# Three of twelve ReLU tiles of each position-bias round move to GpSimd

## The reference

```python
pos = np.arange(S)                                   # S = 576
psi_rel = np.log1p(np.abs(pos[:, None] - pos[None, :]))
psi_i = np.log1p(np.maximum(pos[:, None], 1.0))
x = (psi_rel / psi_i)[..., None]
h = np.maximum(x @ w1 + b1, 0.0)                     # S x S x 32 hidden units
bias = h @ w2                                        # S x S x 8 heads
scores = scores + bias.transpose(2, 0, 1)[None]      # then softmax, times v
```

## Time and profile before

| | |
|---|---|
| timed runs | 1266.56, 1266.70, 1267.24 us; median 1266.7 |
| span of the profiled execution | 1264.6 us |
| bias stage: first VectorE tile to last | 5.02 to 63.84 us |
| first matmul of the attention | 67.56 us |
| DVE busy in the span | 725.5 us (57%), TENSOR_SCALARs at L222: 108 |
| POOL busy in the span | 497.8 us (39%) |
| PE busy in the span | 1219.2 us (96%) |

### The profile page before, as it was taken

How to read it: one execution, slowest core, us unless ns; L and a number is a source line. 1 busy time by engine, 2 the same in 40 slices (tenths; PEclk the granted TensorE clock), 3 DMA queues, 4 the chain that set the end, 5 groups by cost and what they waited for, 6 DMA issues and landing times. The chain is left out here.

```text
span 1264.6 us, 26124 instructions
## 1 busy us (share of the span) xinstructions
PE 1219.2 (96%) x9106; PEld 1096.9 (87%) x9106; DVE 725.5 (57%) x1764; ACT 526.9 (42%) x1188; POOL 497.8 (39%) x588
## 2 busy tenths in 40 slices
PE   6789999999979999999999999999999999999998
PEld 2266777777669999999999999999999999999998
DVE  8977777777779777878778788552112020211111
ACT  6977777777723434344444433212212121212111
POOL 3056666666666424344243444551111111111111
PEclk9989999999999999999999999999999999999999
DMA  5844425252135000000000002340000000000000
GB/s 183 248 146 136 141 95 160 92 179 66 64 95 147 2 1 0 0 0 1 0 0 0 0 0 67 92 117 20 1 19 19 0 19 0 19 0 19 0 19 19
DMA packets 47590, 69.06 MB, mean 55 GB/s; under 512 B 3744, under 2 KB 28480, under 8 KB 47552
## 3 DMA queue, kind: packets, MB, share of 16 engines
q1 hardware_dynamic: 47552, 68.60, 17.4%
HBM read 53.25 MB, written 15.34 MB: 54 GB/s over the span
## 5 line engine op out<-in xcount | busy, mean ns | idle before, releaser
L817 PE MATMUL banks<-x_high,w_high_rest 128*128 128x288 f32 x992 | 293.3, 296 | 0.5 <-PEq L1010 0.5
L818 PE MATMUL banks<-x_low,w_high_rest 128*128 128x288 f32 x992 | 292.8, 295 | 0.0
L819 PE MATMUL banks<-x_high,w_low_rest 128*128 128x288 f32 x992 | 291.8, 294 | 0.0
L1372 DVE TENSOR_TENSOR product<-angle_or_silu,banks 128x288 f32<-128x288 f32 x96 | 43.4, 452 | 312.2 <-PE banks L819 312.2
L1391 POOL TENSOR_TENSOR product_low<-product,product_high 128x288 fp32r<-128x288 f32 x96 | 77.6, 808 | 356.4 <-ACT product_high L1332 356.4
L1190 POOL TENSOR_TENSOR product_low<-product,product_high 128x288 fp32r<-128x288 f32 x128 | 110.4, 863 | 242.5 <-ACT product_high L1070 242.5
L817 PE MATMUL bank<-product_high,w_high_rest 128*128 128x288 f32 x672 | 201.3, 300 | 3.5 <-POOL product_low L1391 2.0
L819 PE MATMUL bank<-product_high,w_low_rest 128*128 128x288 f32 x672 | 197.8, 294 | 0.0
L818 PE MATMUL bank<-product_low,w_high_rest 128*128 128x288 f32 x672 | 197.7, 294 | 0.0
L819 PEld LDWEIGHTS banks<-x_high,w_low_rest 128*128 128x128 f32 x992 | 186.7, 188 | 0.0
L817 PEld LDWEIGHTS banks<-x_high,w_high_rest 128*128 128x128 f32 x992 | 185.9, 187 | 0.7 <-issue 0.7
(11 more groups left out here) (97 smaller groups left out, 2539.4 us busy)
## 6 DMA issues: line engine op xcount, KB each, us to landing
raw_qk<-in_qk SPq DMA_DIRECT2D x32, 576.0 KB, 3.7
bias_scratch<-bias_stage SPq DMA_DIRECT2D x36, 288.0 KB, 3.1
bias<-bias_scratch SPq DMA_DIRECT2D x32, 288.0 KB, 3.1
w_raw<-in_w_out SPq DMA_DIRECT2D x28, 256.0 KB, 2.6
values<-in_v SPq DMA_DIRECT2D x16, 320.0 KB, 4.0
w_raw<-in_w_in SPq DMA_DIRECT2D x16, 256.0 KB, 2.9
out_t<-X SPq DMA_DIRECT2D x7, 576.0 KB, 3.0
w_raw<-in_w_gate SPq DMA_DIRECT2D x12, 256.0 KB, 3.0
```

The source lines that it names most:

```text
L817: nc.tensor.matmul(out, high, x_high, start=start, stop=False)
L818: nc.tensor.matmul(out, high, x_low, start=False, stop=False)
L819: return nc.tensor.matmul(out, low, x_high, start=False, stop=stop)
L1372: dve.tensor_tensor(s[:, :], silu[:, :], val_ps[f % 2][:, 0:NT], ALU.mult).then_inc(s_ready, 1)
```

## The change

GpSimd makes the last tile (j = 3, `POOL_STEP`) of each of the three groups of a round, in VectorE's form. ScalarE makes two tiles of k = 0 instead of three (`ACT_STEPS = [2, 0, 0]`). VectorE makes what is left: one tile of k = 0 (j = 2), three of k = 1, three of k = 2. ScalarE's three copy-outs of a round stay, and so does the shift, whose cut follows `ACT_STEPS`. TensorE has one more wait before each group. GpSimd's rounds are written out one by one; its two prepares come after its tiles of rounds 1 and 2 instead of ahead of everything.

```diff
-    ACT_STEPS = [3, 0, 0]
+    ACT_STEPS = [2, 0, 0]
+    POOL_STEP = STEPS - 1
...
             att.setup(pool)
-            att.prepare(pool, 0, 0)
-            att.prepare(pool, 0, 1)
+            pool.wait_ge(slope_ready, 2)
+            pool.wait_ge(table_in, 16)
+
+            def groups(n, parity, step):
+                for k in range(KINDS):
+                    back = 1 if k == KINDS - 1 else 2
+                    if step >= back:
+                        pool.wait_ge(bias_summed[k], n + 1 - back)
+                        after_waits(pool, pool_passed)
+                    pool.tensor_scalar(hidden[parity][k][POOL_STEP][:, :], table_window(n, k, POOL_STEP),
+                                       slope_of(n, k, POOL_STEP), neg_b1[:, :], ALU.mult, ALU.max
+                                       ).then_inc(pool_hidden[k], 1)
+
+            for n in range(N):
+                groups(n, n % 2, min(n, 2))
+                if n in (1, 2):
+                    att.prepare(pool, 0, n - 1)
...
-                for j in range(ACT_STEPS[0]):
+                for j in range(KINDS):
                     if step > 1 and j == 0:
                         act.wait_ge(bias_summed[0], n - 1)
-                    act.activation(hidden[parity][0][j][:, :], table_window(n, 0, j), ACT.Relu, bias=b1c,
-                                   scale=slope_of(n, 0, j)).then_inc(act_hidden[0], 1)
+                    if j < ACT_STEPS[0]:
+                        act.activation(hidden[parity][0][j][:, :], table_window(n, 0, j), ACT.Relu, bias=b1c,
+                                       scale=slope_of(n, 0, j)).then_inc(act_hidden[0], 1)
                     if step > 0:
                         stage_out(n - 1, 1 - parity, j, step <= 2)
...
-                    for j in range(ACT_STEPS[k], STEPS):
+                    for j in range(ACT_STEPS[k], POOL_STEP):
...
                     pe.wait_ge(dve_hidden[k], n + 1)
+                    pe.wait_ge(pool_hidden[k], n + 1)
```

More of the change, by code:

```diff
@@ L105, in bias_phase @@
     dve_hidden = [sem_of(f"p0_dve_hidden{k}") for k in range(KINDS)]
+    pool_hidden = [sem_of(f"p0_pool_hidden{k}") for k in range(KINDS)]
     bias_summed = [sem_of(f"p0_bias_summed{k}") for k in range(KINDS)]
@@ L109, in bias_phase @@
     dve_passed = sem_of("p0_dve_passed")
+    pool_passed = sem_of("p0_pool_passed")
     scratch = bias_scratch.rearrange("h i j -> i h j")
```

## The result

The changed kernel takes 1315.4 us (median of four runs, 1314.1 to 1316.9) against 1267.0 for the kernel before beside it: ratio 1.0383, 95% interval 1.0368 to 1.0397. The forecast was 1269.7, with a range up to 1276.0. The sign was right and the size was not, by a factor of 16.

What follows compares the result with a forecast made beforehand. VectorE was taken to bound the bias stage, whose length passes fully into the total. Removing 11.77 us of its tiles and adding 14.8 us of collisions gave +3.0 on 1266.7, so 1269.7 us, range 1266.0 to 1276.0.

Steps and rivals of the forecast that it cites:

- What bounds the kernel before, and that the stage's length goes through one for one: Bias stage: VectorE ends each round, 4.41 us, and any change in stage length passes fully into the total.
- outside this stage nothing is changed: After the bias stage: later work keeps its engines and transfers and is only shifted, by the same 3 us.
- The tail of 3.72 us: End of bias stage, from VectorE's last tile to the attention's first matmul: claimed to stay as it is.
- The price of a GpSimd tile, 0.82 us to run: GpSimd's new bias tiles: about 0.82 us each, from 674 ns plus 71 ns for each of two per-partition operands.
- the wait on it: TensorE's new wait for GpSimd's tile in each group: costs nothing, as GpSimd is always half a round ahead.
- rival B: Bias stage: each whole GpSimd instruction blocks VectorE, 0.74 to 0.82 us a tile, giving 1281.6 to 1284.4 us; chance 0.09.
- L = 0.41 between 0.355 and 0.50: VectorE time lost to each of GpSimd's 36 new bias tiles, in us; 14.8 us in all.
- Removed, 11.77 us: VectorE in the bias stage: two tiles fewer a round, 24 at 0.4903 us, saving 11.77 us.
- prepares, 5.50 wherever they stand beside VectorE: GpSimd's two prepares, moved after its rounds 1 and 2: cost VectorE the same 5.50 us as before.
- The rule on the shared port pair: VectorE and GpSimd share a port pair held for a whole instruction; a collision would cost all of GpSimd's instruction.
- C, the prepares: Bias rounds 2 to 5: prepares delay GpSimd's tiles and VectorE stands still, 1 to 4.8 us on top; chance 0.09.
- A, free tiles: Bias stage: VectorE loses nothing to GpSimd's tiles, stage at most 11.8 us shorter, 1254.9 us; chance 0.12.

Runs made afterwards that it cites:

- run 5: Changed kernel plus 16 semaphore increments nobody waits for at the end of VectorE's bias program, restoring its attention loop's address: 1309.1 us, ratio 1.0330.
- run 1: Changed kernel with add in place of max on GpSimd's 36 tiles, both column operands kept: 1280.1 us, ratio 1.0100.
- run 3: Changed kernel with GpSimd's 36 tiles as slope * window * 1.0, leaving out bias and ReLU: 1277.0 us, ratio 1.0072.
- run 11: Changed kernel with add in place of max and 16 unawaited semaphore increments in VectorE's program: 1276.1 us, ratio 1.0079.
- Run 8: Kernel before, first prepare held until late in the bias stage, second prepare and SyncE's two loads moved into the attention programs: 1264.7 us, ratio 0.9985.
- run 4: Changed kernel with only one GpSimd tile a round, still with max; ScalarE makes three and VectorE eight: 1281.0 us, ratio 1.0103.
- run 7: Kernel before, no tile moved, plus 120 unawaited semaphore increments at the end of VectorE's bias program: 1283.6 us, ratio 1.0135.
- run 6: Kernel with one GpSimd max tile a round, plus 8 unawaited semaphore increments in VectorE's bias program: 1270.7 us, ratio 1.0029.

## Why the prediction was wrong, point by point

*What bounds the kernel before, and that the stage's length goes through one for one:* right for the stage, but "outside this stage nothing is changed" was a step that failed, the smaller one of two. VectorE's program lost 16 instructions ahead of its attention loop. Of the 7.0 us lost behind the stage, putting 16 back returned 6.4 in the trace and 6.3 in the medians (run 5). The tail of 3.72 us did not stay either: with the slow clock it was 4.69.

*The price of a GpSimd tile, 0.82 us to run, and the wait on it, "costs nothing":* this is the step that failed by most. I took the duration from rows whose operations are mult and add, and gave the unseen `max` half a sentence in rival B. The tile with max costs 2.28 us alone against 0.83 for add with the same operands (run 1): 1.45 us on each of 36 tiles, 52 in all. With 92 us of tiles and 9 of prepares GpSimd could not be "always half a round ahead": it was always behind, and the wait that I priced at nothing became the one that sets the pace. The attention began 43.5 us later; with add, 6.7.

*What a tile costs VectorE, L = 0.41 between 0.355 and 0.50:* near for one column, too low for the two that the change has. I worked the mean out from VectorE's time from first tile to last, less 84 x 0.4903 for its tiles, 0.27 for the shifts, 5.50 for the prepares and the one wait for TensorE: (63.06 - 41.19 - 0.27 - 5.50 - 0.63) / 36 = 0.43 in run 3, and 0.50 in run 1 and 0.48 in run 11 (65.48 and 64.93 us, waits of 0.64 and 0.53). Single collisions show why: 0.35 without a column, mostly 0.43 with one (run 3) and 0.51 with two (run 1), in steps of 0.08, about the 71 to 81 ns by which GpSimd's tile itself gets longer. So the operands lie inside the time in which VectorE is kept out, the upper bound of the forecast: 36 x 0.50 - 11.77 = +6.2, and a wait of 0.5 to 0.6 us for the k = 2 buffer comes on top, for which the sum had nothing. For the slow tile L is 0.69 to 0.84.

*Removed, 11.77 us; prepares, 5.50 wherever they stand beside VectorE:* no run contradicts them. Run 8 took the prepares away, and the first two rounds became 4.0 shorter; 1.26 of the rest went into the wait for TensorE.

*The rule on the shared port pair, in the Trainium skill ("SBUF — State Buffer", Who interferes with whom):* by it a collision should cost VectorE all of the GpSimd instruction. No run shows this: VectorE lost 0.43 beside a tile that takes 0.745 us alone (0.94 in the collision) in run 3, and 0.69 beside one of 2.8 to 3.8 us in run 4. By these rows they exclude each other for part of the instruction only.

*The rivals:* B had the right place (the unseen `max`), but priced it as port time, 15 to 18 us, and did not ask what a slow GpSimd does to TensorE's new wait. C, the prepares, did not matter beside that, as GpSimd ran without a gap. Nor did C come with fast tiles: in runs 1, 3 and 11 VectorE waited once for its k = 2 buffer, 0.5 to 0.6 us, in round 5 of run 3 and later in the other two. A, free tiles, is out: in run 3, with the cheapest tile, most collisions cost 0.43.

*On the 7 us:* a page of the Trainium skill ("Runtime: NRT & Kernel Launch", Instruction fetch mechanics) says that a taken branch whose target is not in the window held on chip forces a fetch. The trace agrees in kind: gaps of mostly 2.5 to 3.3 us on VectorE, one or two at each of two turns of its loop, and ten more 8 KB packets in the instruction queue in just this time. Which places fit was not measured beyond the shifts tried: none, or one filled up again (no gap), 16 fewer (6 to 8 us), 8 fewer and 120 more (12 us).

*Open:* why max is slow on GpSimd, and whether its extra 1.45 us grow with the tile, as all tiles here were 128x576; why a slow GpSimd tile holds up two VectorE tiles and not one; and what makes the small steps between 358 and 852 us, in which all traces here but run 7's lose 0.6 to 2.8 us against the one of the kernel before, and the 0.4 to 1.7 us that runs 1, 3, 4, 6, 8 and 11 lose in the attention's first 25 us.

## What to carry to other kernels

Before work moves to another engine, ask of that engine's trace for the same operation, not only the same instruction: here TENSOR_SCALAR with add was 0.83 us and with max 2.28. If no row has it, the engine's total with a price three times as high belongs among the rivals, as an engine that becomes the bound. And after any edit compare the parts that were not edited, too: here, with sixteen instructions fewer ahead of a loop, its code was fetched again at its turns (6.3 us), and in another version eight empty ones brought 10.3 us back.

## What the runs showed of the hardware that was not expected

- GpSimd's max and min on float32, 128x576: 2.28 us with two columns, 2.20 with one, 1.65 as the only operation; mult with add or mult: 0.83 and 0.745.
- A column operand costs GpSimd 71 to 81 ns (674, 745, 826 ns for none, one and two, with mult or add; the first writes float32r), and 76 with max (2202 and 2278).
- VectorE's loop in the attention had issue gaps of 6.0 to 7.8 us in all, or of 11.7 to 12.0, or none, by where it lay; the instruction queue showed 29 or 30 packets of 8 KB instead of 19.
- 120 semaphore increments in a row on VectorE, 0.093 us each, delayed the meeting of the engines by 6.3 us in a place where it had some 4 us of idle time.
